# Linear attention and two feed-forward layers on one core: paced early loads, a new order of decay products in round 0, and first steps of rounds 1 and 2 moved behind g

## The reference, cut to what matters

```python
# B, H, S, D = 4, 8, 768, 48
for t in range(S):
    cur = einsum('bhd,bhe->bhde', u[None] * kt, vt)
    y[:, :, t] = einsum('bhd,bhde->bhe', rt, state + cur)
    state = wt[:, :, :, None] * state + einsum('bhd,bhe->bhde', kt, vt)
x = y as (B * S, H * D)              # 3072 x 384
x = ((x @ w_a) * (x @ w_b)) @ w_out  # d_ff 1536
h = x @ w_in2                        # d_ff 2048
out = (maximum(h, 0) + alpha * minimum(h, 0)) @ w_out2
```

## Time and profile before

| | |
|---|---|
| median of 3 runs | 1026.57 us (1026.07 to 1027.17) |
| the profiled execution | 1026.15 us |
| its span in the profile | 1024.4 us |
| TensorE (matmul) busy | 1001.1 us, 98% |
| VectorE busy | 561.9 us, 55% |
| ScalarE busy | 288.4 us, 28% |
| GpSimd busy | 30.2 us, 3% |
| granted TensorE clock | 1.00 |

### The profile page before, as it was taken

The page is one execution under the profiler, slowest core; times in us unless marked ns, Lnnn a source line. Parts: engine busy times, 40 slices in busy tenths (PEclk is TensorE's granted clock), DMA queues, the critical chain, the costliest instruction groups (busy, mean ns, idle before and its releaser), DMA issues.

```text
span 1024.4 us, 29087 instructions
## 1 busy us (share of the span) xinstructions
PE 1001.1 (98%) x12448; PEld 975.5 (95%) x12448; DVE 561.9 (55%) x1166; ACT 288.4 (28%) x604; POOL 30.2 (3%) x28
## 2 busy tenths in 40 slices
PE   5899999999999999999999999999999999999998
PEld 4789999999999999999999999999999999999998
DVE  7587664655646646556432436655454555545554
ACT  3435324224232142241222434222222222122211
POOL 4500200000000000000000000000000000000000
PEclk9999999999999999999999999999999999999999
DMA  6454231311213113020020313010101010101000
GB/s 183 110 158 115 63 81 30 95 42 38 85 30 79 37 30 91 4 61 28 25 60 1 107 64 121 4 47 1 47 1 47 1 46 0 46 0 47 8 17 24
DMA packets 42167, 53.01 MB, mean 52 GB/s; under 512 B 5184, under 2 KB 42048, under 8 KB 42048
## 3 DMA queue, kind: packets, MB, share of 16 engines
q1 hardware_dynamic: 40624, 51.04, 17.6%
q10 hardware_dynamic: 1424, 0.23, 0.2%
HBM read 39.46 MB, written 9.44 MB: 48 GB/s over the span
## 4 chain that ended last, share of the span: by engine, by line
PE 95%; DVE 2%; issue 1%; ACT 1%; DMA 1%; ACTq 0%; SPq 0%; DVEq 0%
PE products L166 17%; PE products L168 16%; PE products L167 16%; PE acc L166 11%; PE acc L168 11%; PE acc L167 11%; PE products L697 6%; PE products L712 1%; PE products L741 1%; PE products L757 1%; PE products L674 1%; PE products L726 1%; DVE f_y L920 1%; DMA w_v<-in_w_dram 1%; DVE k_in L932 0%
## 5 line engine op out<-in xcount | busy, mean ns | idle before, releaser
L166 PE MATMUL products<-x_parts,weights_hi 128*128 128x384 f32 x576 | 200.9, 349 | 2.2 <-DMA x_parts<-f_y 0.5
L167 PE MATMUL products<-x_parts,weights_hi 128*128 128x384 f32 x576 | 194.1, 337 | 0.0
L168 PE MATMUL products<-x_parts,weights_lo 128*128 128x384 f32 x576 | 193.9, 337 | 0.0
L1232 DVE TENSOR_SCALAR leaky_low<-products,leaky_al 128x384 f32<-128x384 f32 x128 | 79.0, 618 | 169.4 <-PE products L168 169.3
L1092 DVE TENSOR_TENSOR g_sb<-a_g,products 128x384 f32<-128x384 f32 x96 | 53.2, 554 | 192.7 <-issue 134.2
L1179 ACT ACTIVATE leaky_g_hi<-leaky_g_sb 128x384 fp32r<-128x384 f32 x128 | 67.3, 526 | 295.0 <-DVE leaky_g_sb L1237 295.0
L515 ACT ACTIVATE g_hi<-g_sb 128x384 fp32r<-128x384 f32 x96 | 50.3, 524 | 259.6 <-DVE g_sb L1092 259.6
L166 PEld LDWEIGHTS products<-x_parts,weights_hi 128*128 128x128 f32 x576 | 108.0, 188 | 7.4 <-issue 3.8
L168 PEld LDWEIGHTS products<-x_parts,weights_lo 128*128 128x128 f32 x576 | 108.2, 188 | 0.0
L167 PEld LDWEIGHTS products<-x_parts,weights_hi 128*128 128x128 f32 x576 | 108.2, 188 | 0.0
L166 PE MATMUL acc<-g_hi,weights_hi 128*128 128x384 f32 x288 | 97.7, 339 | 1.6 <-DVE g_lo L1098 1.0
(11 more groups left out here) (86 smaller groups left out, 1761.9 us busy)
## 6 DMA issues: line engine op xcount, KB each, us to landing
k_in<-in_k_dram SPq DMA_DIRECT2D x16, 336.0 KB, 4.1
r_in<-in_r_dram SPq DMA_DIRECT2D x16, 336.0 KB, 5.8
stage<-in_w_out_dram SPq DMA_DIRECT2D x14, 384.0 KB, 3.2
w_v<-in_v_dram SPq DMA_DIRECT2D x16, 288.0 KB, 4.0
y_dram<-x_in SPq DMA_DIRECT2D x8, 576.0 KB, 3.1
x_in<-y_dram SPq DMA_DIRECT2D x8, 576.0 KB, 4.6
out_dram<-leaky_out_sb SPq DMA_DIRECT2D x7, 576.0 KB, 3.3
stage<-in_w_dram SPq DMA_DIRECT2D x10, 336.0 KB, 4.0
```

What stands on the lines that cost most here:

```text
L166: pe.matmul(out, w_hi, x_hi, start=first, stop=False)
L167: pe.matmul(out, w_hi, x_lo, start=False, stop=False)
L168: return pe.matmul(out, w_lo, x_hi, start=False, stop=last)
L1232: dve.tensor_scalar(self.low[f % 2][:, :], h, 0.0, self.al[:, f:f + 1], ALU.min, ALU.mult).then_inc(self.low_ready, 1)
```

## The change: what it does

- SyncE waits for each of the pieces 0 to 2 to land before it issues the next; in round 0 it also waits for each load of v and each load of r (of round 1) to land before it goes on.
- SyncE issues the loads of w of round 2 ahead of the moves of round 1, not behind them.
- GpSimd no longer does the first steps of round 2. VectorE does them in phase 0 of that round, behind the leaf merges. The first steps of round 1 move on VectorE from phase 0 (ahead of g_sb(0)) to phase 1 (behind g_lo(0)).
- In round 0 VectorE forms the decay product of level 2 ahead of the leaf merge of stream 1, does the second steps of the keys earlier, and the merges of level 2 behind the products of levels 3 to 6.
- Piece 5 is split in slot 1 and not in slot 0; the load of piece 8 moves with it.

```diff
-FIRST_NEW = [5, 6, 7, 9, 10, 11, 13, 15, 16, 17, 18, 18, 18]
+FIRST_NEW = [5, 5, 7, 9, 10, 11, 13, 15, 16, 17, 18, 18, 18]
...
                     if phase == 2:
-                        load_v(n, 0)
-                        load_v(n, 1)
+                        for j in range(2):
+                            load_v(n, j)
+                            if n == 0:
+                                sp.wait_ge(v_loaded[j], 16)
                         if n + 1 < DUOS:
-                            load_r(n + 1, 0)
-                            load_r(n + 1, 1)
+                            for j in range(2):
+                                load_r(n + 1, j)
+                                if n == 0:
+                                    sp.wait_ge(r_loaded[2 + j], 16)
...
                     elif phase == 10:
-                        move_last_unit(n)
+                        if n == 0:
+                            move_last_unit(n)
                         if n + 1 < STAGED_FROM:
                             load_w(n + 1, 0)
                             load_w(n + 1, 1)
+                        if n > 0:
+                            move_last_unit(n)
...
                 for piece in range(STAGES):
                     shared.load_piece(sp, piece)
+                    sp.wait_ge(shared.staged[piece], shared.staged_by[piece])
...
-                def first_step_k(n, j):
-
-                    pool.wait_ge(w_loaded[j], 16 * (n + 1))
-                    pool.wait_ge(k_prepared[j], n + 1)
-                    pool.tensor_tensor(halves(k_in[j], 1, 0), halves(k_in[j], 1, 0), decay(n, j, 1, 1), ALU.mult).then_inc(k_first[j], 1)
-
...
-                for n in range(2, STAGED_FROM):
-                    for j in range(2):
-                        first_step_k(n, j)
-                        step_r(n, j, 0)
...
+                def first_steps(n):
+
+                    for j in range(2):
+                        first_step_k(n, j)
+                        step_r(n, j, 0)
+
...
                             merge_leaf(n, j)
-                        if n == 1:
-                            for j in range(2):
-                                first_step_k(n, j)
-                                step_r(n, j, 0)
+                        if n == 2:
+                            first_steps(n)
                         if n >= STAGED_FROM:
                             first_step_k(n, 1)
                     elif phase == 1 and n > 0:
+                        if n == 1:
+                            first_steps(n)
                         products_of_w(n, 0, 2, range(1, 7))
...
                 products_of_w(0, 1, 1, (1,))
+                products_of_w(0, 0, 2, (2,))
                 merge_leaf(0, 1)
                 step_k(0, 1, 1)
+                step_k(0, 0, 2)
                 merge_level(0, 0, 1)
                 merge_level(0, 1, 1)
-                products_of_w(0, 0, 2, (2,))
-                step_k(0, 0, 2)
+                step_k(0, 1, 2)
                 products_of_w(0, 0, 2, range(3, 7))
-                for step in range(3, BEFORE_TILES):
-                    if step > 3:
-                        attend_early(step)
+                merge_level(0, 0, 2)
+                merge_level(0, 1, 2)
+                for step in range(4, BEFORE_TILES):
+                    attend_early(step)
                     attend(step)
```

## The result

The changed kernel takes 1031.07 us (1029.56 to 1032.22, 7 runs) against 1027.17 us for the kernel before in the same session: ratio 1.004, 95% interval 1.0028 to 1.0051. Two more sessions on other chips gave 1.0041 each. It is slower by 3.9 us, where 1.8 was forecast with 1030.9 as the upper end. The profiled execution took 1032.22 us, the longest of the seven; its span is 1030.4 us, 6.0 more than before.

What follows compares the result with a forecast made beforehand. TensorE was taken as the bound, busy 1001.1 of 1024.4 us. Late keys +3.5, first gate -1.0 and round 2 -0.7 summed to +1.8 us: 1028.4 against the median, range 1025.6 to 1030.9.

Steps and rivals of the forecast that it cites:

- +4.6 at the copies (forecast +3.5): ScalarE's copies of round 0's outputs: predicted to start at 44.3 instead of 40.76, +3.5 us, bounds +1.1 to +6.
- The second key load: Hand-over from round 0 to round 1: predicted to be issued 0.4 us after the first and land at 42.6.
- Rival C: Round 0's paced loads: alone they are as short as the shortest rows, about 1026.0 us; chance 0.17.
- Rival B: Round 0's paced loads: crowding did not cause long landings; alone they take 3.4 and 4.1, 1029.6 to 1031; chance 0.20.
- -1.0 at the first gate: First down of round 1: first steps behind g_lo(0) remove TensorE's 0.97 us idle; -1.0, bounds 0 to -1.1.
- 0.4 us of slack at g_sb(1): VectorE in round 1: products done at 56.3, so g_sb(1), even 1 us earlier than 57.77, has 0.4 to spare.
- Slot 1: Round 1: piece 5's split moves here; cost 0 with some 0.3 us slack, up to 0.5 us if cover is gone.
- -0.7 in round 2: Round 2: early w and first steps on VectorE close TensorE's 0.67 us gap near 129; -0.7, bounds 0 and -0.7.
- rival E: Round 2: the change doesn't do what it says and the 0.67 us stays; +0.7 on any case.
- Round 0's gain "hidden by this wait, all of it": Round 0 reordered on VectorE: 1 to 2 us could go, but the wait for the keys hides it all.
- Rival D: Round 0 to 1: pacing doesn't gate, copies start when TensorE is done; -2.7, 1023.9 us; chance 0.13.

## Why the prediction was wrong

The direction and the path were right: the key loads at 38.07 us for a forecast 38.2, then ScalarE, the moves, the first ups. That the two times agree so closely is partly luck. Piece 1 had landed by 20.09 and not at 21.7; w_out took 3.8 us for 3.0 and v 3.4 and 4.0 for 3.1, and r 3.4 and 3.2 for 3.5. In the two other profiles of the changed kernel the keys go out at 37.66 and 38.90. The range missed the measured time by 0.2 us. Its upper end took the longest landings together with all of the gains, and nothing for the clock. Between the two profiles the sum comes out as +4.6 at the copies (forecast +3.5), +2.6 for the clock (0), -1.2 at the first gate (-1.0), -0.4 around the first ups (0), +1.1 in slots 1 to 3 (0) and -0.7 in round 2 (-0.7), which makes +6.0. The steps that failed, worst first:

*The clock was not in the sum at all.* I wrote that TensorE would idle 3 to 4 us more in 36 to 48 us and gave that no price beyond its length. It idled 6.8 us ahead of the leaf products; the granted clock was 0.66 of full speed in 40 to 60 us, and 18 matmuls stood 0.32 us apart in place of 0.175. That is 2.6 us in this profile and 2.2 and 1.4 in the two others, and filling both idle times gave 2.6 us back. Matmuls at about twice their time are at the 1.2 GHz level in place of 2.4. With the clock held the kernel is 1.9 us over the kernel before (1028.28 against 1026.41), about what the sum without a clock had given. The Trainium skill ("TensorE: Matmul & The Clock Gate", "Part 1: The HAM clock gate") says that the clock is set by how busy the engine has been recently. The runs agree as far as these idle times go: an idle stretch was paid twice. The same section of the Trainium skill puts the penalty of the ramp to full clock under 1% of a typical span, which agrees too (0.25%), but that is more than half of what this change cost.

*The second key load*, taken as 4.0 us, took 5.8 in the profile after. This was no stray: it took 4.7 to 5.9 us in all nine profiles in which SyncE issues the keys behind seven waits, and 3.9 to 4.4 in the nine others. In the three profiles of the changed kernel the copies start 3.6, 4.6 and 4.9 us late, against +3.5; so this term was low by up to 1.4 us, within its own bounds (+1.1 to +6). Rival C, that loads alone are as short as the shortest rows, is false for v (3.4 and 4.0 against 2.8) and true for r (3.4 and 3.2 against 3.3). Rival B, that early loads take 3.4 and 4.1 us alone, comes nearest to the time (1029.6 to 1031), but its reason holds for v at most: r took 3.4 and 3.2, and most of what was missing was the clock. The fit of the Trainium skill ("DMA: Bandwidth & Descriptors", the anatomy of one DMA) gave 2.8 us for 336 KB; the shortest landing of such a load in the profile after was 3.2, so it does not agree. That section of the Trainium skill states the fit for DMAs that GpSimd issues, and these are SyncE's, which the prediction did not say.

*-1.0 at the first gate.* The stall is gone from the changed kernel, and the sum has its 1.2 us there. But the edit alone gives 0.9999: it takes 0.8 us off up to the first level and 0.5 of them come back as a wait at the second down. "What is late next" was asked, and answered by 0.4 us of slack at g_sb(1) that VectorE didn't have.

*Slot 1*, taken as 0 with 0.5 as the price of a lost cover: TensorE waits 0.43 us at 70.58 and 0.27 us at 74.26 in the profile after, the second time behind the load of piece 8 that was to cost nothing. The forecast found the place and trusted a slack of 0.3 us. Putting the split back gains nothing, so the price belongs to the first steps behind g as much as to FIRST_NEW.

*-0.7 in round 2*: right in every row, and in size as far as the timed runs can tell (0.9994, an interval that includes no change). So rival E is false.

*Round 0's gain "hidden by this wait, all of it"*: right. Unpaced, all other parts together give 2.3 us; the order of round 0 alone 1.5 to 2. In the changed kernel the earlier end of round 0 only made TensorE's idle time longer (6.8 us against 1.1 in the kernel before with pacing), and with it the stretch of low clock.

Rival D, that the pacing wouldn't gate, is true of either half of the pacing and false of both.

## What to carry to other kernels

Price a wait in a DMA queue by what is queued behind it and how late that may be: three or four waits cost nothing here and seven cost 0.4% over the kernel before, since the queue had some 3 us to give. When an edit lengthens an idle time of TensorE, add the slow matmuls behind it to the sum. And when work is moved out of the way of one stall, ask what the same engine must deliver next: here half of a gain of 1 us was gone one slot later.

## What had not been expected of the hardware

A TensorE that the profile shows as fully busy can run at half clock: 400 records of 48x48 by 48 in fp32 took 71 ns each, with a granted clock of 0.50 in 50 to 70 us, while 32 matmuls of 128x128 by 384 in the same place held 1.00. With those 32 in the first idle time, the clock fell at about 51 us in one profile, behind 2.5 us of idle for the moved rows, and stayed at 1.00 in the next one of the same kernel; with both idle times filled it stayed at 1.00, and only then did the timed runs gain. The clock column of the profile can read 1.00 over a stretch in which 15 matmuls stand 0.32 us apart.

And of two equal loads of 336 KB issued 0.4 us apart the second took 5.8 us to land and the first 3.5, after SyncE had waited for all the loads before them. The second was late in all nine profiles in which SyncE issues the keys behind the seven waits (4.7 to 5.9 us), while with the waits behind v and r only, and the same 0.4 us between the two, it took 4.1. Why is open.
